# Token rows scattered in three rounds into one DRAM region per expert, each expert's rows loaded and turned beside the expert before

## What is computed

```
# 1. a gated linear attention: per head a complex state of 48 x 48, decayed and rotated at each step
for t in range(S):
    S_re, S_im = decay(a[t]) * (S_re + i S_im);  S_re += outer(k[t], v[t]);  y[t] = q[t] @ S_re
x = y as [1536, 384]
# 2. a mixture of 8 experts, at most capacity = 384 tokens each, in order of the tokens
logits = x @ w_gate;  expert = argmax(logits);  gate = softmax(logits)[expert]
token i gets place pos = number of earlier tokens with the same expert, and is kept if pos < capacity
out[i] = gate[i] * (relu(x[i] @ w1[expert]) @ w2[expert])   if kept, else 0
# 3. a dense MLP, hidden width 2048:  h = out @ w_in;  (max(h,0) + alpha*min(h,0)) @ w_out
```

## Time and profile before

| | us |
|---|---|
| median of three runs (513.11 to 514.43) | 514.22 |
| the profiled execution | 512.74 |
| its span in the trace | 510.8 |
| PE busy | 448.6 (88%) |
| DVE, ACT, POOL busy | 353.6, 262.1, 40.1 |
| PE idle before line 1314 in all experts, for DVE's low part of the hidden tile | 0.9 |
| a weight chunk's load, from issue to landing, median | 3.6 |

### The profile page before, as it was taken

One profiled execution on the slowest core, in us unless ns is written; L12 is line 12 of the kernel. 1 busy time (PEld: TensorE's weight loads), 2 busy tenths in 40 slices (PEclk: granted clock), 3 DMA queues, 4 the chain that ended last, 5 costly groups with the idle time before them and its releaser, 6 DMA issues.

```text
span 510.8 us, 9796 instructions
## 1 busy us (share of the span) xinstructions
PE 448.6 (88%) x3648; PEld 406.4 (80%) x3648; DVE 353.6 (69%) x555; ACT 262.1 (51%) x419; POOL 40.1 (8%) x50
## 2 busy tenths in 40 slices
PE   0458999999910999999999999999999999999995
PEld 0237778999800899999999988999989999899985
DVE  3999999943160777777777767887747877488751
ACT  4999894844440666666666643333343333333312
POOL 3000000000148400000000000000030000300003
PEclk9979999999965799999999999999999999999999
DMA  8990001000034976666766652333333233210001
GB/s 314 422 376 3 4 3 3 4 3 3 3 124 158 337 226 201 196 185 189 221 202 197 187 187 88 98 99 104 99 118 106 94 121 97 98 57 0 1 0 66
DMA packets 27150, 63.76 MB, mean 125 GB/s; under 512 B 7894, under 2 KB 9430, under 8 KB 27100
## 3 DMA queue, kind: packets, MB, share of 16 engines
q1 hardware_dynamic: 25564, 58.34, 35.5%
q0 software_dynamic: 1536, 4.74, 2.4%
HBM read 58.28 MB, written 4.76 MB: 123 GB/s over the span
## 4 chain that ended last, share of the span: by engine, by line
PE 77%; ACT 9%; issue 3%; DVE 3%; POOL 3%; DMA 2%; DVEq 1%; SPq 0%; POOLq 0%; ACTq 0%
PE banks L1306 16%; PE banks L1304 16%; PE banks L1305 16%; PE banks L1314 8%; PE banks L1086 4%; PE banks L1315 4%; PE banks L1110 2%; POOL rows_by_slot L390 2%; ACT L422 2%; PE banks L1072 2%; PE banks L1113 2%; PE banks L1041 2%; PE banks L1075 2%; DMA th<-a_im_rows 1%; PE banks L1298 1%
## 5 line engine op out<-in xcount | busy, mean ns | idle before, releaser
L957 DVE TENSOR_TENSOR w_lo<-raw_early,w_hi 128x768 fp32r<-128x768 f32 x84 | 80.1, 956 | 30.4 <-ACT w_hi L591 29.4
L636 ACT ACTIVATE g_hi<-g_all 128x512 fp32r<-128x512 f32 x48 | 30.3, 632 | 118.4 <-DVE g_all L1014 116.0
L591 ACT ACTIVATE w_hi<-raw_early 128x768 fp32r<-128x768 f32 x84 | 70.3, 843 | 33.4 <-PE banks L1315 32.8
L1304 PE MATMUL banks<-w_hi,g_hi 128*128 128x384 f32 x192 | 65.1, 339 | 0.5 <-DVE g_lo L1016 0.5
L1306 PE MATMUL banks<-w_hi,g_lo 128*128 128x384 f32 x192 | 65.0, 339 | 0.0
L1314 PE MATMUL banks<-h_hi_lo,w_hi 128*128 128x448 f32 x192 | 64.0, 379 | 1.1 <-DVE h_hi_lo L977 0.9
L1305 PE MATMUL banks<-w_lo,g_hi 128*128 128x384 f32 x192 | 64.9, 338 | 0.0
L1016 DVE TENSOR_TENSOR g_lo<-g_all,g_hi 128x512 fp32r<-128x512 f32 x48 | 33.3, 693 | 44.3 <-ACT g_hi L636 44.3
L1304 PE MATMUL banks<-ys_hi,w_hi 128*128 128x512 f32 x144 | 56.1, 389 | 1.2 <-DVE ys_lo L991 1.2
L1306 PE MATMUL banks<-ys_hi,w_lo 128*128 128x512 f32 x144 | 57.1, 397 | 0.0
L1305 PE MATMUL banks<-ys_lo,w_hi 128*128 128x512 f32 x144 | 56.8, 394 | 0.0
(11 more groups left out here) (146 smaller groups left out, 916.5 us busy)
## 6 DMA issues: line engine op xcount, KB each, us to landing
raw_early<-weights SPq DMA_DIRECT2D x84, 384.0 KB, 3.6
raw_late<-weights SPq DMA_DIRECT2D x28, 384.0 KB, 2.9
xq<-q_rows SPq DMA_DIRECT2D x3, 776.0 KB, 16.8
xq<-rows_by_slot SPq DMA_DIRECT2D x12, 194.0 KB, 4.1
kk<-k_rows SPq DMA_DIRECT2D x3, 768.0 KB, 18.2
vv<-v_rows SPq DMA_DIRECT2D x3, 768.0 KB, 19.6
aa<-a_re_rows SPq DMA_DIRECT2D x2, 768.0 KB, 10.7
th<-a_im_rows SPq DMA_DIRECT2D x2, 768.0 KB, 12.1
```

Of the source, the lines that this page charges most:

```text
L591: A(wh[:, slot, :], raw[slot], ACT.Copy).then_inc(w_hi, 1)
L636: A(gh[:, c % GBUF, :], gg[:, c % GBUF, :], ACT.Copy).then_inc(g_hi, 1)
L957: TT(wl[:, slot, :], raw[slot], wh[:, slot, :].bitcast(F32), ALU.subtract).then_inc(w_lo, 1)
L1304: MM(o, lhsT=whi, rhs=mhi, start=first, stop=False)
```

## The change

- The list sorted by expert is replaced by a DRAM region per expert of 1536 rows. Tokens of batch 0 are written downwards from the region's middle, those of batch 1 upwards, so a token's place depends only on the tiles of its own batch before it, and no total is needed.
- Routing is done in three rounds, of 6, 4 and 2 row tiles (ROUNDS), each with choose (DVE), rank (PE) and place (DVE). The scatters of a round follow its place, and at most four scatters are in flight.
- A window of 384 rows from each region holds the expert's tokens. Rows of a region that no token fills must be zero, so SP writes zeros to 384 rows of each of the eight regions (from the middle up), after the first frame's decay transfers. The source is a zeroed SBUF tile read by broadcast, in pieces of 192 numbers.
- After the last round SP loads the window of expert 0 in three tiles, then weight chunks 6 and 7 of the first expert, then the windows of experts 1 and 2. Later windows are loaded in the experts' loop, each behind a wait until an earlier expert's window buffer is free (four buffers).
- PE turns two tiles of 128 rows of the next expert's window inside each expert, behind its outputs 1 and 4; ACT and DVE split them at steps 3 and 6. Only expert 0 has its two tiles turned ahead of the first matmul. A third tile would be turned on the wide path.
- Gates and final slots are computed by DVE in six parts within expert 0, scattered to DRAM by POOL in 12 small scatters, each waiting for the one before, and read back once. Rows in xq are 384 numbers wide.
- Some x_transpose and tile_logits calls move forward in PE's list, with ACT's copies, and two ranking steps are put in.
- The experts' outputs use four banks in turn instead of five.

```diff
+                if f == 1:
+                    for e in range(E):
+                        sp.dma_start(xs_dram[e * REGION + MID:e * REGION + MID + CAP, :].rearrange(
+                            "(p t) (a c) -> p (t a) c", t=WT, a=UW // ZERO),
+                            nothing[:, None, :].to_broadcast([P, WT * (UW // ZERO), ZERO])).then_inc(zeroed, 16)
...
+            sp.wait_ge(windows, 1)
+            start_rows = [window_row(e) for e in range(FIRST)]
+            for i in range(IN_FLIGHT):
+                sp.wait_ge(scattered[i], 16 * (NT // IN_FLIGHT))
+            for t in range(WT):
+                sp.dma_start(win[:, 0, t, :], window_rows(start_rows[0], t, 1)[:, 0, :]).then_inc(first_dma[t], 16)
             for i in range(AHEAD, RING):
                 sp.dma_start(raw[i], w_in[i, :, :]).then_inc(w_dma[i], 16)
-
-            sp.wait_ge(scattered, 16 * NT)
-            for r in range(0, NT, LOAD_ROWS):
-                sp.dma_start(orow[:, r:r + LOAD_ROWS, :],
-                             xs_dram[r * P:(r + LOAD_ROWS) * P, :].rearrange("(t p) w -> p t w", p=P)
-                             ).then_inc(row_dma[r // LOAD_ROWS], 16)
+            for e in range(1, FIRST):
+                load_window(e, start_rows[e])
...
+            for e in range(1, E):
+                if FIRST - 1 < e + FIRST - 1 < E:
+
+                    sp.wait_ge(used, USED_FREE + RING * max(e + FIRST - WB, 0))
+                    load_window(e + FIRST - 1, window_row(e + FIRST - 1))
...
                     load_chunk(RING * e + i, RING * e + (i + 1 - RING), i)
+                if e == E // 2:
+                    sp.wait_ge(meta_scattered, 16 * NT)
+                    sp.dma_start(meta[:, :, :], meta_dram.rearrange("(t p) w -> p t w", p=P)).then_inc(meta_dma, 16)
...
+            pool.wait_ge(zeroed, 16 * E)
+            for r, (n0, n1) in enumerate(ROUNDS):
+                pool.wait_ge(routed, r + 1)
+                for t in range(B * n0, B * n1):
+                    if t >= IN_FLIGHT:
+                        pool.wait_ge(scattered[t % IN_FLIGHT], 16 * (t // IN_FLIGHT))
+                    pool.indirect_dma_start(xs_dram, bass.IndirectOffsetOnAxis(ap=slots_i[:, t:t + 1], axis=0),
+                                            xq[:, t * UW:(t + 1) * UW], None).then_inc(scattered[t % IN_FLIGHT], 16)
+            pool.wait_ge(bases, 1)
...
+            pool.wait_ge(meta_ready, 1)
+            for t in range(NT):
+                if t > 0:
+                    pool.wait_ge(meta_scattered, 16 * t)
+                pool.indirect_dma_start(meta_dram, bass.IndirectOffsetOnAxis(ap=comp_i[:, t:t + 1], axis=0),
+                                        meta_src[:, t, :], None).then_inc(meta_scattered, 16)
...
+            act.wait_ge(logits_made, XT_FREE + NT)
+            for i in range(FIRST):
+                split_hi(i, i, 1)
...
                         split_hi(RING * e + (i + AHEAD), (i + AHEAD) % RING, e + (1 + (i + AHEAD) // RING))
+                        if i in NEXT_AT and e + 1 < E:
+                            window_hi(e + 1, NEXT_AT.index(i))
...
+            def choose(r):
+
+                n0, n1 = ROUNDS[r]
+                T = slice(B * n0, B * n1)
+                n = B * (n1 - n0)
+                dve.wait_ge(logits_made, XT_FREE + B * n1)
+                if r == 0:
+                    dve.wait_ge(zeroed, 16 * E)
+                source = LB[:, T.start * E:T.stop * E].rearrange("p (t e) -> p t e", e=E)
+                if r + 1 < len(ROUNDS):
+                    dve.tensor_copy(logit[:, T, :], source).then_inc(logits_out, 1)
+                    dve.wait_ge(logits_out, r + 1)
+                    source = logit[:, T, :]
+                then(dve.tensor_reduce(top[:, T], source, AX_X, ALU.max))
+                then(TT(rt[:, 0, T, :], source, wide(top[:, T], n), ALU.is_equal))
+                then(TT(rt[:, 0, T, :], rt[:, 0, T, :], prior[:, None, :].to_broadcast([P, n, E]), ALU.mult))
+                then(dve.tensor_reduce(best[:, T], rt[:, 0, T, :], AX_X, ALU.max))
...
+                    STT(one_hot[:, T.start + 1, :], rt[:, 0, T.start + 1, :], best[:, T.start + 1:T.stop], sign[:, 1, :],
+                        ALU.is_equal, ALU.mult).then_inc(onehot, 1)
+                dve.wait_ge(onehot, r + 1)
+                for m in range(n0, n1):
+                    TT(before[:, m + 1, :, :], before[:, m, :, :], one_hot[:, B * m:B * m + B, :], ALU.add
+                       ).then_inc(prefixed, 1)
+                    if m + 1 < n1:
+                        dve.wait_ge(prefixed, m + 1)
...
+            def place(r):
+
+                n0, n1 = ROUNDS[r]
+                T = slice(B * n0, B * n1)
+                dve.wait_ge(ranked, r + 1)
+                TT(rt[:, 0, T, :], RK[r][:, 0:B * (n1 - n0) * E].rearrange("p (t e) -> p t e", e=E),
+                   one_hot[:, T, :], ALU.mult).then_inc(ranks_read, 1)
+                dve.wait_ge(ranks_read, r + 1)
+                then(dve.tensor_reduce(slot[:, T], rt[:, 0, T, :], AX_X, ALU.add))
+                TT(slots_i[:, T].rearrange("p (n b) -> p n b", b=B), slot[:, T].rearrange("p (n b) -> p n b", b=B),
+                   sign[:, None, :, 0].to_broadcast([P, n1 - n0, B]), ALU.mult).then_inc(routed, 1)
...
             mask_scores(2, 1)
+            choose(0)
             mask_scores(2, 2)
+            place(0)
             mask_scores(2, 3)
             mask_scores(2, 4)
             mask_scores(2, 5)
+            choose(1)
             mask_scores(2, 6)
             mask_scores(2, 7)
-
-
-            steps = [0]
-
-            def then(ins):
-                steps[0] += 1
-                ins.then_inc(route_steps, 1)
-                dve.wait_ge(route_steps, steps[0])
-
-            dve.wait_ge(logits_made, XT_FREE + NT)
-            dve.tensor_copy(logit[:, :, :].rearrange("p t e -> p (t e)"), LB[:, 0:NT * E]).then_inc(logits_out, 1)
-
-            def wide(ap):
-                return ap[:, :, None].to_broadcast([P, NT, E])
-
-            dve.wait_ge(logits_out, 1)
-            top, total, gate, keep, rank, slot = (rs[:, i, :] for i in range(6))
-            start = top
-            then(dve.tensor_reduce(top, logit[:, :, :], AX_X, ALU.max))
+            place(1)
+
+
+            choose(2)
+            place(2)
...
+                        if e == 0:
+                            gate_part(i)
+                        if i in NEXT_AT and e + 1 < E:
+                            window_lo(e + 1, NEXT_AT.index(i))
...
+            def rank(r):
+
+                n0, n1 = ROUNDS[r]
+                to = RK[r][:, 0:B * (n1 - n0) * E]
+                if r == 1:
+                    pe.wait_ge(state_out, U_FREE + 6 * (NF - 1) + 2)
+                pe.wait_ge(ranks_read, r)
+                pe.wait_ge(prefixed, n1 - 1)
+                MM(to, lhsT=ones[:, :], rhs=before[:, n0:n1, :, :].rearrange("p n b e -> p (n b e)"), start=True, stop=False)
+                pe.wait_ge(onehot, r + 1)
+                MM(to, lhsT=upto[:, :], rhs=one_hot[:, B * n0:B * n1, :].rearrange("p t e -> p (t e)"),
+                   start=False, stop=True).then_inc(ranked, 1)
...
+            def window_T(e, t):
+                if e > 0:
+                    pe.wait_ge(row_lo, NTILES * e + t)
+                tile_T(e, t).then_inc(row_T, 1)
...
+                        if i in NEXT_FROM and e + 1 < E:
+                            window_T(e + 1, NEXT_FROM.index(i))
```

395 lines of the change are left out of this document (239 added, 156 removed).

## The result

| | before | after |
|---|---|---|
| median, four runs each | 513.99 us (513.11 to 514.43) | 526.19 us (524.17 to 529.16) |
| the profiled execution, its span | 512.74, 510.8 | 525.50, 523.8 |

The ratio is 1.0245, with a 95% interval from 1.0224 to 1.0266: the change makes the kernel 12 us slower. The forecast was 507.2, with a range from 499 to 517. The profiled execution lies 19.8 us above the 505.7 that the sum gave for it.

What follows compares the result with a forecast made beforehand. PE was taken as full except for a 33.3 us hole between attention and experts. Gain 19.9 less 2.0 (clock, DVE), 5.0 (transposes) and 5.9 (fill) gave 7.0 us: 507.2 from a median of 514.22, range 499 to 517.

Steps and rivals of the forecast that it cites:

- last router matmul later by PE's new order: End of attention: an extra logits tile and two ranking pairs in PE's full row delay the last logits by 1.4 us.
- zero fill: stall and clock: Attention: angles queued behind a 16 us fill stall PE 4.9 us, then a low clock costs 1.0; 5.9 in all.
- scatters beside the attention: Rounds one and two during attention: DVE's extra work falls in idle time, POOL is free by 144.3; no cost.
- last router to first expert matmul: Handover to experts: routing 2.6, second scatter 1.5, landing 2.6, load to turned tiles 5.06, first matmul 0.2 us.
- turns, clock and DVE in the experts: Experts: 14 tile turns in PE's full row cost 5.0 us, low clock 1.5 and DVE's gate steps 0.5 in expert 0.
- weight chunks and gates in SP's queue: Experts: late weight loads behind a window wait, and the gates' scatters, were both costed at 0.
- rival 4: Routing rounds don't overlap, so the last queues behind ten scatters: 12.7 us, 519.9; chance 0.12 together with rival 3.
- the bunching: Experts 2 to 5's weight loads queue behind a window wait; ACT 1.6 us late, covered by about 3 us, cost 0.
- Rival 2: Experts: the bunched weight loads show, adding 6.4 us for 513.6; chance 0.11.
- at no cost: List of items priced at nothing: POOL's added constants, the gates' one-at-a-time scatters, fewer banks of expert output.
- Rival 3: Zero fill at 84 ns per row lasts 32 us and stalls 20.9: 523.2; chance 0.12 together with rival 4.
- signs of being wrong: Angles before 80, fill over 23 us, PE waiting over 3 us inside experts, or round three finding POOL busy.

Runs made afterwards that it cites:

- e10_all_mended: Kernel after with fills behind the second decay hop, scatters paced, window loads behind weight chunks, gates' wait behind the last expert's chunks; 504.80 us.
- e8_chunks_first: Kernel after with each later window load put behind the expert's eight weight chunks in SP's queue instead of ahead of them; 520.71 us.
- e15_long_train: Kernel before with twelve added back-to-back scatters of 64 B rows behind the 9th output tile, over the end of the attention; 532.56 us, one run.
- e11_paced: Kernel after with round one's scatters each waiting for the previous landing and round two's held until the last logits; 515.66 us.
- e6_one_in_flight: Kernel after with one scatter in flight instead of four, each waiting for the one before to land; 522.90 us.
- e9_trains: Kernel before with added trains of 64 B row scatters in GpSimd's idle time, in attention and experts, read by nothing; 515.70 us.
- e1_fill_late: Kernel after with the eight zero fills behind the second decay hop in SP's queue instead of the first; 516.35 us.

## Why the prediction was wrong

The forecast's terms beside what they measured, in us:

| term | forecast | measured |
|---|---|---|
| last router matmul later by PE's new order | 1.4 | 1.4 (e10_all_mended: 141.96 - 140.57) |
| zero fill: stall and clock | 5.9 | 6.9 (100.61 - 93.75); 6.1 to 8.0 in other kernels |
| scatters beside the attention | 0 | 11.1 (159.93 - 148.31, less 0.5 ahead of them) |
| last router to first expert matmul | 11.96 | 12.08 |
| turns, clock and DVE in the experts | 7.0 | 7.4 (e8_chunks_first: 136.57 - 129.15) |
| weight chunks and gates in SP's queue | 0 | 6.0 (142.54 - 136.57) |
| the span behind the experts (209.2, 207.8 before), and the execution's own time over its span | 0 | 1.2 |

Three lines hold the miss: 11.1, 6.0 and 1.2 of the 19.8, with 1.5 from the sizes of the others.

**The step that failed** is the one that places the scatters: "DVE's own extra work there (about 2 us per round) falls in its idle time. The last four scatters of round two start at about 139 and leave POOL at 144.3". It asked whether POOL and DVE had room for them, and took for granted that PE doesn't feel POOL; the cost was put at nothing, and the runs showed 11.1 us. The twelve scatters of before stand in the hole, where PE does nothing. The trace of before does have scatters at the same spacing beside full matmuls, two trains of four output scatters in the last MLP:

```profile
374.46 0.96 POOL L399 DMA_INDIRECT out_rows<-xq,tok_slot  x1 [202.86 <-ACT xq L645]
375.73 0.96 POOL L399 DMA_INDIRECT out_rows<-xq,tok_slot  x1 [0.30 <-issue]
...
370.00:378.00 8.00, 8.00 (x40) 6.95 (x39) 2.20 (x3) 3.41 (x6) 2.94 (x3) 1.00 0.20 76
```

PE is busy for all of the 8 us. So that trace even spoke for a cost of zero, but only beside five large matmuls per us; the product groups of the attention run over thirty, and no row showed a scatter beside those. A term without a row of its like needs a price range; it had none, and rival 4, which did speak of the rounds, looked only at when they could run.

**The step that was mis-sized** is the bunching: "ACT is 1.6 late, and the hidden tile that it holds up has about 3 us until PE wants it". ACT was not 1.6 but 4.35 us late in expert 1 and waited nine times. Rival 2 gave 6.4 as the price, and SP's queue cost 6.0 in all; that the two agree is chance. By the pitches of e8_chunks_first the bunching took 2.4 us in experts 0 to 2, and expert 4, where the gates' wait stands, lost 3.6. The gates stood in the list "at no cost": "12 x 3.1 = 37 us of POOL, from the middle of expert 0 to expert 3". They took 57.3 us (188.97 to 246.25), a median of 4.2 from issue to landing, and so ran into expert 4. And the wait was costed by who wants its result, not by what is queued behind it on SP: expert 7's window and expert 5's chunks, for 13.0 us.

**What was right.** The fill: the angles reached DVE at 84.65, forecast 84.8. It moved 285 GB/s at a DMA share of 0.92; over 16 engines that is 19.4 B/ns, or 40 ns for a 768 B row, where 42 had been taken. The 42 was lucky in part: it rests on 65 ns for a written 1552 B row, but the page of before has 1536 packets for 4.74 MB on the scatters' queue, 3.1 KB on average, so a scatter's packets weren't single rows. An estimate by the Trainium skill (DMA: Bandwidth & Descriptors, "Specifications" and "Why small descriptors are slow") had given 12.4 us of fill, 32 ns a row, and 1.3 us of stall; the trace has 40 ns a row and a stall of 4.45 us before PE's angle sums, so here the measurement decides against so small a price per packet. The hole (11.96 against 12.08), the pitch of an undisturbed expert (16.57, forecast 16.9; before 15.98 in the mean of experts 1 to 6, so two turns cost 0.6), and the two tiles turned ahead of the first matmul all came out nearly as written. The clock at the start of expert 0 was priced at 1.5: PE works from 172 to 178 at 0.55, which is 2.7 us, and expert 0 takes 19.0 to 19.4 us even in the mended kernels.

**The rivals.** Rival 3, the slower one, had the fill as its mechanism; the time came out slower by another. Rival 4 didn't happen: the first scatter of round three starts 2.8 us behind the last logits, with POOL free. One of the forecast's signs of being wrong did come, PE waiting inside experts by more than 3 us in all (by the windows it is idle for 3.9 in experts 1, 2 and 4). A forecast of 0.82 for faster rested on the sizes of named steps, and left nearly nothing for work that is placed where no row shows its like.

## What to carry to other kernels

Ask of work that is moved beside other work not only whether its engine is free, but whether the trace shows the two side by side, with the same kind of instruction; if it doesn't, give the pair a price range, or try it alone first. Cost a wait by everything that is queued behind it on its engine, and put loads with a far due time behind those with a near one. And a train of indirect scatters next to dense small matmuls wants gaps: with a 0.55 us memset behind each it cost 0.8 us here, without gaps 11.1 us in the kernel after and 18.2 in e15_long_train.

## What the runs showed of the hardware

- Indirect scatters issued by GpSimd every 1.27 us can all but stop TensorE: 45 matmuls in 14.2 us in e15_long_train, at a DMA share of 0.03. Its next post comes 0.4 to 3 us behind the start of the last one. The stalls stay when bytes, targets, source tile, waits for landings or the place of code loads are changed; scatters 1.78 us apart cost 0.8 us over a whole stretch, scatters 2.8 us apart nothing in e11_paced and 0.8 us in e6_one_in_flight.
- It begins in some of PE's program and not in all of it. Twelve scatters in the experts and six beside single product groups (e9_trains), and four beside the last MLP (before), held nothing; all stalls began in a group of the small state-and-value products (112*64 and 128*64 in the rows) close behind another. Why is not known.
- A stall of 5 us can be followed by up to 18 us at a granted clock near 0.54 although PE is busy throughout (e1_fill_late, 133 to 151 us), or by 6 us at 0.72 (the kernel after). The same kernel then differs by 6.6 us and more from run to run (513.95 to 520.52).
- SP's own queue is held while it issues: the eight fills took 10.87 us to issue, 0.7 for each of the first two and 1.9 for the last.
